# The first keys and receptances come over ScalarE's DMA queue instead of SyncE's

## What is computed

```python
def _attn_ref(r, k, v, w, u):              # 2 batches, 8 heads, 768 tokens, head size 48
    for t in range(S):
        cur = np.einsum('bhd,bhe->bhde', u[None] * kt, vt)
        y[:, :, t] = np.einsum('bhd,bhde->bhe', rt, state + cur)
        state = w[None, :, :, None] * state + np.einsum('bhd,bhe->bhde', kt, vt)

def _moe_ref(x, domain_probs, w1, w2):     # 1536 tokens, width 384, 4 experts of 1024
    p = domain_probs / (domain_probs.sum(-1, keepdims=True) + 1e-09)
    for e in range(E):
        h = np.maximum(x @ w1[e], 0.0)
        out += p[:, e:e + 1] * (h @ w2[e])

def _moe2_ref(x, w_in, w_out):             # 384 to 2048 and back
    h = x @ w_in
    return (h * (1.0 / (1.0 + np.exp(-1.702 * h)))) @ w_out
```

## Time and profile before

| | us |
|---|---|
| median of 3 runs | 644.05 |
| lowest and highest | 643.66, 644.24 |
| the profiled execution | 644.99 |
| its span, first to last instruction | 643.1 |

### The profile page before, as it was taken

How to read it: one execution, slowest core, us unless ns; L and a number is a source line. 1 busy time by engine, 2 the same in 40 slices (tenths; PEclk the granted TensorE clock), 3 DMA queues, 4 the chain that set the end, 5 groups by cost and what they waited for, 6 DMA issues and landing times.

```text
span 643.1 us, 9503 instructions
## 1 busy us (share of the span) xinstructions
PE 637.1 (99%) x3914; PEld 531.8 (83%) x3914; DVE 220.4 (34%) x370; ACT 202.7 (32%) x419; POOL 169.0 (26%) x165
## 2 busy tenths in 40 slices
PE   8999999999999999999999999999999999999998
PEld 6999888888888888888888888888888888888886
DVE  7887653212121212121212121213433333333332
ACT  3754443332222211222211223222643333333223
POOL 6444310342242302242402245421760000000000
PEclk8999999999999999999999999999999999999999
DMA  8846440006000311000310000220000010001001
GB/s 325 306 157 216 153 169 25 29 3 244 1 0 1 152 45 50 1 1 0 118 79 1 0 1 1 73 123 1 2 1 0 1 49 1 0 2 49 1 1 49
DMA packets 8723, 39.08 MB, mean 61 GB/s; under 512 B 1505, under 2 KB 1633, under 8 KB 7393
## 3 DMA queue, kind: packets, MB, share of 16 engines
q1 hardware_dynamic: 8672, 38.40, 15.8%
HBM read 36.01 MB, written 2.38 MB: 60 GB/s over the span
## 4 chain that ended last, share of the span: by engine, by line
PE 97%; DVE 1%; issue 0%; DMA 0%; ACT 0%; DVEq 0%
PE bank L1064 46%; PE bank L1090 31%; PE bank L1106 15%; PE bank L1138 2%; PE bank L1180 1%; PE bank L1183 1%; PE bank L1172 1%; PE bank L1157 1%; PE bank L1188 0%; DVE q_r_mid L796 0%; PE bank L1175 0%; PE bank L1196 0%; DMA wu_sb<-wu_rows 0%; DVE w_pow L777 0%; DVE q_a_t L891 0%
## 5 line engine op out<-in xcount | busy, mean ns | idle before, releaser
L1064 PE MATMUL bank<-x_hi,w_hi 128*128 128x512 f32 (+1 forms) x456 | 172.4, 378 | 0.0
L1064 PE MATMUL bank<-x_lo,w_hi 128*128 128x512 f32 (+1 forms) x456 | 172.3, 378 | 0.0
L1064 PE MATMUL bank<-x_hi,w_lo 128*128 128x512 f32 (+1 forms) x456 | 172.3, 378 | 0.0
L853 DVE SCALAR_TENSOR_TENSOR h_lo<-bank,h_hi 128x512 fp32r<-128x512 f32 (+1 forms) x104 | 67.5, 649 | 257.0 <-ACT h_hi L683 257.0
L683 ACT ACTIVATE h_hi<-bank 128x512 fp32r<-128x512 f32 (+1 forms) x104 | 58.7, 564 | 286.8 <-PE bank L1064 286.8
L605 POOL TENSOR_TENSOR w_lo<-staging,w_hi 128x384 fp32r<-128x384 f32 x80 | 82.3, 1041 | 173.4 <-ACT w_hi L653 173.4
L1090 PE MATMUL bank<-h_hi,w_hi 128*128 128x512 f32 (+1 forms) x312 | 117.4, 376 | 0.0
L1090 PE MATMUL bank<-h_lo,w_hi 128*128 128x512 f32 (+1 forms) x312 | 116.3, 373 | 0.0
L1090 PE MATMUL bank<-h_hi,w_lo 128*128 128x512 f32 (+1 forms) x312 | 116.3, 373 | 0.0
L1064 PEld LDWEIGHTS bank<-x_lo,w_hi 128*128 128x128 f32 x456 | 85.8, 188 | 15.9
L1064 PEld LDWEIGHTS bank<-x_hi,w_hi 128*128 128x128 f32 x456 | 85.8, 188 | 15.9
(11 more groups left out here) (80 smaller groups left out, 435.0 us busy)
## 6 DMA issues: line engine op xcount, KB each, us to landing
staging<-weights SPq DMA_DIRECT2D x10, 1536.0 KB, 9.0
rkv_in<-rkv_n SPq DMA_DIRECT2D x10, 640.0 KB, 4.5
rk_in<-rk_t SPq DMA_DIRECT2D x12, 512.0 KB, 5.5
staging<-weights SPq DMA_DIRECT2D x4, 768.0 KB, 10.5
p_bc<-p_normalised SPq DMA_DIRECT2D x4, 768.0 KB, 4.5
out<-p_bc SPq DMA_DIRECT2D x9, 256.0 KB, 2.1
rkv_in<-rkv_n SPq DMA_DIRECT2D x2, 448.0 KB, 5.9
u_bc<-u_rows SPq DMA_DIRECT2D x1, 192.0 KB, 9.3
```

The costliest lines, as they stand in the source:

```text
L853: dve.scalar_tensor_tensor(h_lo[:, slot, 0:size], hid, 0.0, h_hi[:, slot, 0:size].bitcast(F32), ALU.max, ALU.subtract).then_inc(sem["hlo"], 1)
L1064: last = pe.matmul(bank[:, HID[j % 2], 0:tokens.stop - tokens.start], w[:, k, :], xs[c][:, k, tokens], start=(n == 0), stop=(n == 3 * KT - 1))
```

## The change

The load of chunk 0's keys and receptances leaves SP's queue and becomes the first instruction of ACT's program; it signals the same semaphore. In SP's program `wu_sb` is still first, and all that stood behind the moved transfer stands one place further ahead.

```diff
@@ block.sync @@
-            for c in range(ALONE):
+            for c in range(1, ALONE):
                 load_rk(c)
             for c in range(ALONE):
                 load_rkv(c)
@@ block.scalar @@
         def _(act):
+
+            act.dma_start(rk_in[:, 0], rkT[0]).then_inc(s_rk[0], 16)
             act.wait_ge(sem["zero"], 2)
 
             act.activation(bank[:, KV_BANK, 0:PAIRS * SW], zeros[:, :].to_broadcast([P, PAIRS * SW]), ACT.Copy).then_inc(sem["q_psum"], 1)
```

## The result

The changed kernel takes 649.27 us (median of 10 runs, 645.70 to 650.71) against 644.02 for the kernel before (10 runs, 643.66 to 644.82): the ratio is 1.0068, 95% interval 1.0056 to 1.0080. It is 5.2 us slower, and its times are not one cluster.

| changed kernel, 10 runs | us | mean clock |
|---|---|---|
| four runs | 645.70, 646.25, 646.31, 646.63 | 0.997 |
| three runs | 649.21, 649.32, 649.43 | 0.991 to 0.992 |
| three runs | 650.26, 650.50, 650.71 | 1.000, 1.000, 0.989 |

What follows compares the result with a forecast made beforehand. PE, busy 637.1 of 643.1 us, was taken as the bound, its start waiting on the decays' load. SP 0, ACT 0, chunk 0 earlier 0 and decays late +1.6 turned the 644.05 median into 645.65, range 643.8 to 647.0.

Steps and rivals of the forecast that it cites:

- SP's sooner issues: SP's queue behind the moved transfer: everything issued 0.45 us sooner, gain on the path 0.
- ACT's issue: Front of ACT's program: the added DMA issue takes 0.45 us, covered by 0.68 idle before L636; cost 0.
- the rival of a transfer stuck behind it: ACT's start: moved transfer goes out after the table load at 2.08, L793 0.8 late, 644.85; chance 0.05.
- The decays held by the sharing of the engines: Kernel start: decays' load shares DMA engines with the 512 KB transfer and lands 1.6 us late; chance held in full 0.42.
- The marks named for it: Chain after the change: decays' DMA about 3.5 us, scans start at 4.4, first L1138 at 8.2.
- the 0.2 taken off for small packets that slip in first: Decays' delay: 0.2 us subtracted because some small packets are in before the first big one.
- The upper bound: Decays' landing: they wait until the big transfer has landed at 4.71, against 2.73; 2.0 us late.
- The clock, once more: PE's lead: late decays lengthen the pause, half clock covers both stretches; 1.6 + 1.54 more, 647.2; chance 0.08.
- The sum: Whole kernel: SP 0, ACT 0, chunk 0 earlier 0, decays late +1.6; profiled execution 646.6, median 645.65.
- may as well fall once, but earlier, which costs the same: PE's clock around the lead: one earlier fall to half clock, at the same cost as now.
- The rival in which the fall does not come: PE's lead: the clock fall at 11.20 may not come, 1.54 us gained, 642.5; chance 0.07.
- The range: Whole kernel's time: 643.8 to 647.0 us, leaving out the faster case and part of the slowest, about 0.15.

Runs made afterwards that it cites:

- the slow profile: Changed kernel run again with no edit, profiled in its runs near 650.8 us; median 650.37 us (6 runs).

## Why the prediction was wrong

**Right: the mechanism up to PE's first attention matmul.** SP's sooner issues 0; ACT's issue 0.40 (taken as 0.45), its L638 released by the scans; the table load behind the DMA, so the rival of a transfer stuck behind it falls. The decays held by the sharing of the engines: taken as +1.6, measured +1.57 in the profile. The marks named for it came out as 4.40 (forecast 4.4) for the scans and 8.20 (8.2) for the first attention matmul, and the profiled execution at 646.63 (646.6). That it fits to the hundredth is luck: the next two profiles with the same transfers have +1.36 and +1.06, and the 0.2 taken off for small packets that slip in first was a guess. The upper bound, chunk 0 landed at 4.71, was in truth 4.93; SP's next transfer, which joins 0.45 us sooner, is the likely reason, not tried by itself. The 108 packets against 97 show that the two queues are served in turn, about one for one. By the Trainium skill, DMA: Bandwidth & Descriptors, Queues, rings and completion order, an engine takes turns between queues, which fits; the nine to seventeen descriptors that it names as typical for one turn would have let all of an engine's eight small rows pass at once, and that did not happen.

**Wrong: the last step, "The clock, once more".** The sum took the clock's part of the change as nothing; the rival that priced it got a chance of 0.08 and 1.54 more, 647.2. It was the likely case: 11 of the 16 runs of the changed kernel in the two comparisons. Two things failed in it. First its size: I priced one more stretch over L1180, L1183 and L1188. What runs at half clock in the slow profile is all of the lead, whose four steps grow by 0.92 + 0.81 + 0.92 + 0.81 = 3.46 us, and the small matmuls up to 21 us. The groups at 649.2 and 650.5 lie 3.0 and 4.2 above the 646.3 of the first four runs. Second its chance: I took the pause of 1.6 us as something that moves the fall about, and gave "may as well fall once, but earlier, which costs the same" without a number. The runs with idle work show that 0.7 is enough. I also dismissed w_rev and the transposes because they are not in the chain; but they end PE's pause, and so bear on its clock. The profile showed PE with pauses of only 0.28 and 0.56 between 1.4 and 7.8 us; I did not treat that as a margin.

**Wrong too: reading the profiled fall as a fixture.** The half-clock stretch at 11.20 of before is in the profiled execution and, by the mean clock, in a part of the runs only (6 of 17, 8 of 29 and 2 of 16 in the three comparisons of the experiments). That execution was 0.94 over the median, as the prediction noted; this is where it came from. The rival in which the fall does not come had thus nothing to gain on the median, where it was priced at 642.5: most runs of before were already without it.

**The range** was drawn from one execution's sum. The sum was right for that execution, and the quantity asked for was a median over executions which fall into groups.

What stays open: whether a given run loses the clock. The same program, with nearly the same chain up to 8 us, gives all three groups. Pauses of 1.61 and 1.80 us stand in two profiles of it, and the clock fell at 12.53 in one and at 7.45 in the other. No experiment here sets which.

## What to carry to other kernels

A transfer moved to a second queue does not come for free beside a small one that starts the chain: they share the DMA engines packet by packet, and the small one lands nearly as late as the large one (4.30 and 4.93 us here). And at the head of a kernel, treat an added pause of PE as a risk to its clock, and time several runs, since one profile can miss the loss: here a start late by 0.45 us was harmless, and one late by 0.7 cost over six times its own length in the median. Where a wait there must grow, lengthen the warming work with it, as the two runs with 12 matmuls did.

## What the runs showed that I had not expected

The time of a changed front was two effects of different kinds: 1.0 to 1.6 us of lateness, in each of the three profiles with these transfers, and some 3 to 4.5 us of clock, in 11 of 16 runs. The mean clock of a run does not sort them alone: 1.000 stands both for the best runs of the kernel before (643.4 to 644.6) and for runs at 650.3 to 650.8. And two transfers of 512 KB issued 0.12 us apart on two queues share the engines as well: chunk 0's, the later of them, took 5.10 us to land in place of 3.9.
